# Second-layer output of the last token group with tokens on the partitions

## The reference

```
w   = softmax(weight_gen) over 7 taps           # 8 heads
x   = sum over the 7 taps of w * shifted x      # causal, per head of 24 numbers
h   = x @ w_in1;  g = max(h, 0)**2;             x = g @ w_out1     # first layer, "RELU2"
h   = x @ w_in2;  g = h * sigmoid(1.702 * h);   out = g @ w_out2   # second layer, "GELU"
```

## Time and profile before

| | us |
|---|---|
| median of 3 runs | 1127.59 (1127.42 to 1127.87) |
| the profiled execution | 1127.36 |
| its span, first to last instruction | 1125.6 |
| PE busy | 1119.6 |
| DVE busy | 719.8 |
| ACT busy | 664.4 |

### The profile page before, as it was taken

How to read it: one execution, slowest core, us unless ns; L and a number is a source line. 1 busy time by engine, 2 the same in 40 slices (tenths; PEclk the granted TensorE clock), 3 DMA queues, 4 the chain that set the end, 5 groups by cost and what they waited for, 6 DMA issues and landing times.

```text
span 1125.6 us, 25367 instructions
## 1 busy us (share of the span) xinstructions
PE 1119.6 (99%) x9857; PEld 929.2 (83%) x9857; DVE 719.8 (64%) x875; ACT 664.4 (59%) x708; POOL 3.2 (0%) x9
## 2 busy tenths in 40 slices
PE   9999999999999999999999999999999999999998
PEld 7888888888888888888888888888888888888887
DVE  8885684846758467584765847558485684845332
ACT  6874756656565555656556656465655656555544
POOL 1000000000000000000000000000000000000000
PEclk9999999999999999999999999999999999999999
DMA  6510101010010100101001010010101001000001
GB/s 195 154 64 15 46 8 45 14 49 14 6 43 14 49 14 9 43 11 49 14 12 44 8 49 14 15 44 7 47 14 46 17 6 44 14 14 15 1 4 27
DMA packets 78945, 36.48 MB, mean 32 GB/s; under 512 B 58125, under 2 KB 75533, under 8 KB 78793
## 3 DMA queue, kind: packets, MB, share of 16 engines
q1 hardware_dynamic: 78076, 35.14, 11.7%
q10 hardware_dynamic: 844, 1.01, 0.3%
HBM read 24.30 MB, written 6.29 MB: 27 GB/s over the span
## 4 chain that ended last, share of the span: by engine, by line
PE 99%; DVE 0%; ACTq 0%; ACT 0%; issue 0%
PE hidden L918 41%; PE acc L937 21%; PE acc L929 20%; PE acc L933 10%; PE hidden L922 5%; PE acc L985 1%; PE hidden L819 0%; PE acc L1014 0%; ACT L509 0%; PE acc L873 0%; ACTq L386 0%; DVE attn L323 0%; PE acc L876 0%; PE acc L882 0%; PE acc L881 0%; PE acc L880 0%
## 5 line engine op out<-in xcount | busy, mean ns | idle before, releaser
L918 PE MATMUL hidden<-xin,win 64*128 64x512 f32 x4064 | 698.8, 386 | 0.0
L929 PE MATMUL acc<-g_hi,wout 64*128 64x512 f32 x2032 | 541.6, 386 | 0.0
L918 PEld LDWEIGHTS hidden<-xin,win 64*128 64x128 f32 x4064 | 473.7, 184 | 78.6 <-issue 0.2
L674 DVE TENSOR_TENSOR g_lo<-gate,g_hi 128x1024 fp32r<-128x1024 f32 x256 | 313.4, 1224 | 231.5 <-ACT g_hi L534 226.5
L929 PEld LDWEIGHTS acc<-g_hi,wout 64*128 64x128 f32 x2032 | 373.9, 184 | 39.1
L933 PE MATMUL acc<-g_lo,wout 64*128 64x512 f32 x1016 | 311.7, 386 | 0.0
L937 PE MATMUL acc<-g_lo,wout 64*128 64x512 f32 x1016 | 311.6, 386 | 0.0
L937 PE MATMUL acc<-g_hi,wout 64*128 64x512 f32 x1016 | 311.3, 386 | 0.0
L517 ACT ACTIVATE first<-hidden 128x1024 f32<-128x1024 f32 x128 | 131.5, 1027 | 198.9 <-PE hidden L918 198.8
L530 ACT ACTIVATE gate<-hidden 128x1024 f32<-128x1024 f32 x128 | 131.2, 1025 | 194.4 <-PE hidden L918 193.3
L933 PEld LDWEIGHTS acc<-g_lo,wout 64*128 64x128 f32 x1016 | 186.7, 184 | 20.3 <-DVE g_lo L674 1.1
(11 more groups left out here) (98 smaller groups left out, 353.8 us busy)
## 6 DMA issues: line engine op xcount, KB each, us to landing
window<-x SPq DMA_DIRECT2D x14, 960.0 KB, 4.8
out<-work SPq DMA_DIRECT2D x360, 16.0 KB, 1.4
raw<-term SPq DMA_DIRECT2D x336, 16.0 KB, 1.8
work<-moe_w_out SPq DMA_DIRECT2D x8, 384.0 KB, 4.3
probs<-weight_gen SPq DMA_DIRECT2D x1, 1568.0 KB, 9.9
work<-moe_w_in SPq DMA_DIRECT2D x3, 512.0 KB, 4.5
work<-moe_w_in SPq DMA_DIRECT2D x4, 256.0 KB, 4.1
work<-moe_w_in SPq DMA_DIRECT2D x7, 128.0 KB, 4.4
```

What stands on the lines that cost most here:

```text
L674: nc.vector.tensor_tensor(g_lo[:, s.k, :], gate[:, s.k, :], g_hi[:, s.k, :], ALU.subtract).then_inc(g_ready, 1)
L918: return nc.tensor.matmul(hidden[:, s.k, chunk, :], w[rows, wi, odd if place else even], xt[rows, xi, :], start=start, stop=stop)
L929: return nc.tensor.matmul(acc[b.acc][:, 0, :], wo[rows, 2 * b.j + c, wcols], g_hi[rows, b.k, c * N:(c + 1) * N], start=start, stop=False)
```

## The change

For the last group alone, the second layer's output products have the tokens on the PSUM partitions. The stationary operand is now a 128-token piece of `g_hi` or `g_lo`; the moving operand is `w_last`, which holds for each chunk the 192 hi columns and beside them the 192 lo columns. A product with `g_hi` streams all 384 columns into one bank (hi and lo sums beside each other), one with `g_lo` the first 192. Four token tiles take four banks: `last_sums(t)` is bank `t // 2` of `acc[RELU2]` for even `t` and of `acc[GELU]` for odd `t`. 

- `last_products` takes the place of `both_products` where `b` is one of the last group's GELU pairs (six calls, `j` = 0 to 5). Before its first product into `acc[GELU]` (`t` = 1, `j` = 0) it waits for `out_turned` and `out_summed` of the group before.
- `output_last` takes the place of `output_product` for `j` = 6 and 7. For `j` = 7, tiles 2 and 3 go through `apart` into banks of `hidden`, with 192 columns in each product.
- ACT fills `w_last` in the buffer of the first layer's `wout` (four times three copies, `last_weights`, after the pairs n+7 to n+10).
- At the end ACT copies the lo sums of each tile and DVE adds the hi sums; for tiles 2 and 3 DVE adds the `hidden` bank on top. Three stores follow: tiles 0 and 1 and then tile 2 on ACT's queue, tile 3 on SP's. The copies to SBUF, `fold_eye`, the products against it and the transposes at the end are gone.
- In the last group's `split`, the columns are reordered so that a token tile is 128 columns in a row.

```diff
@@ PE: what is issued for one of the six pairs
+            def last_products(s, b):
...
+                def pair_of_streams(t_low, t_high, g, start=False):
+                    n = 2 * D if g is g_hi else D
+                    for c in range(2):
+                        for rows, t in ((low, t_low), (high, t_high)):
+                            last = nc.tensor.matmul(last_sums(t)[:, 0:n], g[rows, b.k, c * N + P * t:c * N + P * t + P],
+                                                    w_last[rows, 2 * b.j + c, 0:n], start=start and c == 0, stop=False)
+                    return last
+
+                for m in range(4):
+                    hidden_half(low, 0, m, start=m == 0)
+                    hidden_half(high, 1, m, start=m == 0)
+                hidden_tail(low, 0, X_REST)
+                hidden_tail(high, 1, X_TWIN).then_inc(tile_done, 1)
+                output_free(b, False)
+                pe.wait_ge(w_last_in, 3 * (b.j // 2 + 1))
+                pe.wait_ge(g_used, b.n)
+                pe.wait_ge(hi_done[b.layer], in_layer(b))
+                for t in range(2):
+                    if begin and t == 1:
+                        pe.wait_ge(out_turned, GROUPS - 1)
+                        pe.wait_ge(out_summed, GROUPS)
+                    pair_of_streams(t, 2 + t, g_hi, start=begin)
+                    if t == 0:
+                        pe.wait_ge(g_ready, b.n + 1)
+                    last = pair_of_streams(t, 2 + t, g_lo)
+                last.then_inc(tile_done, 1)
+                pe.wait_ge(tile_done, 2 * b.n + 1)
+                for m in range(4):
+                    hidden_half(high, 0, m, stop=m == 3)
+                    last = hidden_half(low, 1, m, stop=m == 3)
+                last.then_inc(hidden_done, 1)
+                pe.wait_ge(tile_done, 2 * b.n + 2)
+                for t in range(2):
+                    pair_of_streams(2 + t, t, g_hi)
+                    last = pair_of_streams(2 + t, t, g_lo)
+                last.then_inc(g_used, 1)
@@ PE: j = 6 and 7
+            def by_tokens(b, t, g, stop=False):
+                for c in range(2):
+                    src = g[:, b.k, c * N + P * t:c * N + P * t + P]
+                    n = 2 * D if g is g_hi else D
+                    last = nc.tensor.matmul(last_sums(t)[:, 0:n], src, w_last[:, 2 * b.j + c, 0:n], start=False,
+                                            stop=stop and c == 1)
+                return last
+            def apart(b, t, g):
+                for c in range(2):
+                    src = g[:, b.k, c * N + P * t:c * N + P * t + P]
+                    last = nc.tensor.matmul(final_sums(t), src, w_last[:, 2 * b.j + c, 0:D],
+                                            start=g is g_hi and c == 0, stop=g is g_lo and c == 1)
+                    if g is g_hi:
+                        nc.tensor.matmul(final_sums(t), src, w_last[:, 2 * b.j + c, D:2 * D], start=False, stop=False)
+                return last
+            def output_last(s):
+                end = s.j == PAIRS - 1
+                pe.wait_ge(hi_done[s.layer], in_layer(s))
+                for t in range(TG):
+                    if end and t >= 2:
+                        apart(s, t, g_hi)
+                        apart(s, t, g_lo).then_inc(tokens_summed, 1)
+                    else:
+                        by_tokens(s, t, g_hi)
+                        if t == 0:
+                            pe.wait_ge(g_ready, s.n + 1)
+                        last = by_tokens(s, t, g_lo, stop=end or t >= 2)
+                        if end:
+                            last.then_inc(tokens_summed, 1)
+                if not end:
+                    last.then_inc(g_used, 1)
@@ ACT
+            def last_weights(part):
+                rows = slice(4 * part, 4 * part + 4)
+                src, dst = wout[GELU][:, rows, :], w_last[:, rows, :]
+                act.wait_ge(g_used, FIRST_N + 16 * ROUNDS + 4)
+                nc.scalar.activation(dst[:, :, 0:D], src[:, :, 0:D], ACT.Copy).then_inc(w_last_in, 1)
+                nc.scalar.activation(dst[:, :, D:D + P], src[:, :, 2 * P:2 * D], ACT.Copy).then_inc(w_last_in, 1)
+                nc.scalar.activation(dst[:, :, D + P:2 * D], src[:, :, D:2 * P], ACT.Copy).then_inc(w_last_in, 1)
...
+                    for m, t in enumerate((2, 3, 0, 1)):
+                        if m == 0:
+                            act.wait_ge(g_used, s.after)
+                        if m >= 2:
+                            act.wait_ge(tokens_summed, t + 1)
+                        nc.scalar.activation(last_low[:, t, :], last_sums(t)[:, D:2 * D],
+                                             ACT.Copy).then_inc(low_copied, 1)
...
+            act.wait_ge(token_out, 4)
             act.dma_start(last_dram[:, 0:2, :], last_tokens[:, 0:2, :]).then_inc(out_done, 16)
+            act.wait_ge(token_out, 5)
+            act.dma_start(last_dram[:, 2, :], last_tokens[:, 2, :]).then_inc(out_done, 16)
@@ DVE
+                    for m, t in enumerate((2, 3, 0, 1)):
+                        dve.wait_ge(low_copied, m + 1)
+                        to = last_tokens if t < 2 else last_most
+                        nc.vector.tensor_tensor(to[:, t, :], last_sums(t)[:, 0:D], last_low[:, t, :],
+                                                ALU.add).then_inc(token_out, 1)
+                    for t in range(2, TG):
+                        dve.wait_ge(tokens_summed, t + 1)
+                        dve.wait_ge(token_out, TG)
+                        nc.vector.tensor_tensor(last_tokens[:, t, :], final_sums(t), last_most[:, t, :],
+                                                ALU.add).then_inc(token_out, 1)
@@ SP
+            sp.wait_ge(token_out, 6)
+            sp.dma_start(last_dram[:, 3, :], last_tokens[:, 3, :]).then_inc(out_done, 16)
```

More of the change, by code:

```diff
@@ L152, in build @@
         sums_of = sb("sums_of", [P, TG * H])
-        last_main = first[:, 0, 0:N]
-        last_rest = first[:, 0, N:2 * N]
+        w_last = wout[RELU2]
         last_tokens = first[:, 1, 0:TG * D].rearrange("p (t d) -> p t d", d=D)
+        last_low = first[:, 0, 0:TG * D].rearrange("p (t d) -> p t d", d=D)
+        last_most = gate[:, 0, 0:TG * D].rearrange("p (t d) -> p t d", d=D)
         last_dram = out.rearrange("(p g t) d -> g p t d", p=P, t=TG)[T // TG - 1]
@@ L460, in _ @@
             pool.wait_ge(zeroed, 2)
-            nc.gpsimd.tensor_tensor(fold_eye[:], ident[:, 0:HALF], ident[:, HALF:P], ALU.add).then_inc(consts, 1)
         def hidden_of(s):
@@ L489, in half_turned, with last_sums, final_sums @@
             return acc[GELU if part else RELU2][:, h, 0:2 * P].rearrange("p (t q n) -> p t q n", t=2, n=QUAD)
+        def last_sums(t):
+            return acc[GELU if t % 2 else RELU2][:, t // 2, 0:2 * D]
+        def final_sums(t):
+            return hidden[:, 0, t - 2, 0:D]
         def by_column(plane):
@@ L874, in output_product @@
[L874 to L882, removed]
@@ L975, in both_products, with hidden_half, hidden_tail @@
                 main_lo(high, 1, stop=end).then_inc(g_used, 1)
+            def last_products(s, b):
+                w, xt, last_lo = win[s.layer], xin[s.x], tail[s.layer]
+                even, odd = (slice((2 * s.j + c) * P, (2 * s.j + c + 1) * P) for c in range(2))
+                by_main = ((W_HI, X_HI), (W_HI, X_LO), (W_LO, X_HI), (W_REST_HI, X_REST))
+                begin = b.j == 0
+                def hidden_half(rows, chunk, m, start=False, stop=False):
+                    wi, xi = by_main[m]
+                    place = 1 - chunk if wi == W_REST_HI and rows == high else chunk
+                    return nc.tensor.matmul(hidden[:, s.k, chunk, :], w[rows, wi, odd if place else even],
+                                            xt[rows, xi, :], start=start, stop=stop)
+                def hidden_tail(rows, chunk, xi):
+                    return nc.tensor.matmul(hidden[:, s.k, chunk, :], last_lo[rows, s.j, :], xt[rows, xi, :],
+                                            start=False, stop=False)
+                def pair_of_streams(t_low, t_high, g, start=False):
[33 more added lines that the diff above has]
+                last.then_inc(g_used, 1)
@@ L1039, in run @@
                         behind.append(s)
-                        if len(behind) > 2:
+                        if len(behind) > 2 and behind[0].layer == GELU and by_tokens_at_last(behind[0]):
+                            last_products(s, behind.pop(0))
+                        elif len(behind) > 2:
                             both_products(s, behind.pop(0), opened)
@@ L1057, in _ @@
                 run(a_round(i), behind_round(i))
[L1058 to L1073, removed]
+            left = run(closing(ROUNDS), behind_round(ROUNDS))
+            for b in left:
+                output_last(b)
 _INS = ["x", "weight_gen", "moe_w_in", "moe_w_out", "moe2_w_in", "moe2_w_out"]
```

51 lines of the change are left out of this document (19 added, 32 removed).

## The result

The changed kernel takes 1129.8 us (median of 22 runs, 1128.17 to 1130.61) for 1127.86 us before (22 runs beside it on the same chip, 1127.4 to 1129.16): a ratio of 1.0014, 95% interval 1.0008 to 1.002. That is 0.9 to 2.3 us slower. By the 0.2% bound (2.3 us) it is no change, as forecast, though the interval reaches up to that bound, and not for quite the reasons forecast: the difference of the medians is +1.9 us where my sum has +0.2. The median lies inside the stated range (1125.6 to 1130.5) and beyond rival A's own (to 1129.3).

A forecast was written before the change was run, and what follows sets the result against it. PE, busy 99% of the span, was taken to bound the kernel. Calls 0.00, wait +2.32, end -1.40 and store -0.70 gave +0.22 us on 1127.36, so 1127.8 us for the median, range 1125.6 to 1130.5.

The forecast's parts named there:

- my sum: Whole kernel: 0.00 + 2.32 - 1.40 - 0.70 = +0.22 us on the profiled execution's 1127.36.
- rival A: Whole kernel: the time comes out as summed, 1127.8 us, own range 1126.4 to 1129.3; chance 0.57.
- The wait: Call for n+14, before tile 1: PE stands still 2.32 us until DVE has added the halves; nothing gives it back.
- Does the clock fall in it? ... I cost it at nothing: PE's standstill in n+14: clock stays full, as for 2.70 us after PE's last product in the trace; cost nothing.
- Rival F: Call for n+14: the clock drops in the wait; one call at 1.2 GHz costs up to 4.3 us, 1132; chance 0.05.
- The six calls at 0.00: Six calls with new products: 9 x 0.2266 + 8 x 0.173 + 8 x 0.110 = 4.306 us each, as before.
- the short slot is held by the load: 192-column products: streaming would take 0.093 us, but the least distance of two loads makes it 0.110 us.
- rivals B: Last group's output products: short streams are slow by themselves, 72 x 0.22 = 15.8 us, 1143.6; chance 0.12.
- D: Last group's output products: short slots are stream-bound at 0.085 us, giving 1126.0; chance 0.12.
- E: Last group's output products: loads count with their full record, 0.184 us, adding 6.0 us, 1133.8; chance 0.06.
- The end: After PE's last product: last store issued 1.40 us earlier, landing in 2.2 us, a further -0.7.
- What hid the calls' ACT copies: ACT's copies into `w_last`, 1.85 us in each of four pairs: ACT's free time hides them, costing nothing.

## Why the prediction was right, and where it was not

- **The wait: right.** The place, the releaser and the length came out (2.40 us for 2.32), and taking it away gave back all of it. Reading which of DVE's instructions the new wait hangs on, and that nothing of the change moves them, was enough.
- **"Does the clock fall in it? ... I cost it at nothing": this step failed.** The clock fell in 15 of the 22 runs, and the median is therefore a run in which it fell: +1.4 us between the medians of the two levels (1128.55 and about 1130.0). The row that I went by, 2.70 us at full clock after PE's last product, is real, but it is one execution, and nothing ran on PE afterwards, so a loss that shows only when PE works again could not be in it. Rival F got 0.05, and its mechanism came in more than half of the runs; its price of 4.3 us was too large, since only 3.4 us ran at half clock, which loses 1.6 us. That the median still lies in the stated range is owed to the range's upper end, which left room for a brief clock drop that the sum did not price: all fifteen of these runs lie beyond rival A's 1129.3.
- **The six calls at 0.00: right in the term that I worried about, wrong in the one I took as given.** The output products take 2.23 us for 2.26, the short slot is held by the load, and with that rivals B, D and E fall. Those 2.23 us leave 0.106 us for a short slot behind the long slots' 0.173; the transposes' row gives the same when it is read as the `fold_eye` row was, (1.78 - 0.19) / 15, and not the 111 ns that I wrote. The Trainium skill (TensorE: Matmul & The Clock Gate, Back-to-back issue gap) would have had a short slot at some 89 ns, an estimate between its two points. The trace does not agree. But the nine hidden slots of a call grew by 0.012 us each, +0.074 us net in a call and +0.37 over the five calls behind the wait. I had taken their 0.2266 us as a property of 512 columns; it is one of the company that they keep.
- **The end: right in size, -2.0 for -2.24.** One link is late: I had tile 2's add out of the way 0.19 us ahead of tile 3's. It began 0.48 us after the end of tile 1's and so held tile 3's, which began 0.14 us after PE's last product and not 0.04, by 0.1 us. The last store took 2.4 us for 2.2.
- **The sum.** 0.37 + 2.40 + 0.20 - 2.0 = +1.0 at full clock, from the profiled execution before, and +1.4 in most runs. That execution, 1127.36, lies 0.5 us below the median of the 22 runs before, so the sum of the two, 2.4, is 0.5 above the measured difference. Between medians it is +0.7 at full clock (1128.55 for 1127.86), 2.1 with the clock lost, and +1.9 for all 22 runs.
- **What hid the calls' ACT copies held.** No wait of PE on `w_last` shows, and the kernel without the wait is 1.8 us faster than before, ratio 0.9984: what the change was worth all along, less the wait.

## What to carry to other kernels

When new work first writes a buffer that others still read, look for work that does not need it and put that ahead: here reordering two calls turned +0.14% into -0.16%. Price a standstill of the tensor engine twice, for its length and for the clock behind it, and don't take a single quiet stretch of one trace as proof that the clock holds. Short streams are paid for by their weight load: halving 192 columns to 96 here took a product from about 0.106 us to 0.095, and not by the 0.04 us of its stream.

## What the runs showed of the hardware

- **After the same standstill the clock falls in some runs and not in others.** With 2.2 us without a product by the bracket (2.4 by the slots) the mean clock was 0.998 in 15 of 22 runs of the changed kernel, in one of its two later runs, and in 5 of 7 of the kernel with the wait alone; in the two with shorter and longer streams, one run each, it was 1.000. With 3.4 us it was 0.998 or 0.997 in 9 of 9; with 0.67 us or none it was never below 0.999 (44 runs, four kernels with 11 each).
- **Where it falls.** In the three traces that have it, the clock reads 1.00 in the standstill and 0.50 for about 3.4 us behind it, from some 1.3 us after PE's restart on in two of them and from the restart itself in the one with the longer wait. It can fall with PE idle too: at the end of the kernel before it did.
- **A 512-column slot depends on its neighbours:** 0.2266 us beside 512 columns, 0.230 beside 384, 0.239 where every second pair of output products streams 192, 0.245 where it streams 96.
- **Two adds of DVE in a row, from different PSUM banks, stood 0.39 to 0.48 us apart** with no semaphore that the runs could blame; with the longer wait they stood 0.10 us apart.
- **The last store of 96 KB landed in 2.2 to 2.4 us** where it was issued 0.26 to 0.33 us behind another one, and in 1.7 us in the one trace where it was issued 0.51 us behind.
